# Blocks of the row maximum at moving slots, another set of units for GpSimd, and a held-back last tile

## The chip, the cores and the metric

The kernel runs on one core of a Trainium2 chip. Its metric is the device time of one execution in microseconds (us). The core has five engines, each with its own instruction queue: TensorE (PE in the rows; its weight loads are PEld) for matmuls, VectorE (DVE), ScalarE (ACT), GpSimd (POOL), and SyncE (SP), which here issues every DMA. The engines wait for each other only through semaphores. A matmul writes to PSUM, 8 banks of 2 KB for each of 128 partitions; the rest lies in SBUF.

## The reference

```
q: (4, 8, 1152, 64)   q_pool = mean of pairs of rows of q          -> (4, 8, 576, 64)
scores = q_pool @ k.T / 8;  attn = softmax(scores);  x = attn @ v   -> 2304 tokens x 512
h = x @ w_in (512 x 2048);  g = h * sigmoid(h);  y = g @ w_out
a = y @ w1;  b = y @ w2 (512 x 1024);  out = ((a * b) @ w3) @ w_out2
```

All in float32. The kernel makes each product from two parts of each operand, a high half rounded to the matmul's format and a low half (the value minus its high half): hi x hi + hi x lo + lo x hi, three matmuls for one.

## The kernel before

**Attention.** 32 heads are worked on as 16 pairs (index p in the code). The two heads of a pair lie on partitions 0 to 63 and 64 to 127, and TensorE issues their 64-row matmuls by twos, which run side by side. The text calls two such matmuls a slot. The keys of a pair are 9 chunks of 128, the queries two halves of 288, so a pair has 18 units u: 0 to 8 (half A) and 9 to 17 (half B). n = 18 p + u counts units through. For each unit TensorE computes the transposed scores (score_t, four slots, the last of which subtracts the row maximum), ScalarE takes the exponential twice (line 526 gives the high half pH, line 531 or 533 the full value), and VectorE (line 735) or GpSimd (line 442) subtracts the one from the other: this is the low half of the unit, pL. For a unit in POOL_UNITS it is made by GpSimd, from a copy in SBUF; else by VectorE, straight from PSUM. Then TensorE multiplies with v, two units later: values(n, 0) and values(n, 1), three slots each. So a unit has ten slots.

score_t(n) overwrites the PSUM banks of unit n - 2: it waits for the low half of unit n - 2, if VectorE makes it, and otherwise only for ScalarE's second exponential. values(n, 0) always waits for the low half of unit n.

**The maximum.** The row maximum of the next pair is found under the units of this one. The scores in their other layout are made in 15 blocks (score_max, line 925: three slots, 384 columns wide), VectorE reduces each (take_max, line 701). From pair 1 on, all blocks use one double bank, so a block waits for take_max of the block before. Blocks stand in units 17 and 0, 2 to 9 and 11 to 15; units 1, 10 and 16 have none. At the end reduce_max, negate and nine small matmuls (turn_max, line 936, in unit 17) turn the maximum.

**The order in a unit of TensorE**, written out by hand: scores; values(n - 3, 1); the block; values(n - 2, 0). In units 2 and 11 the block comes ahead of the scores, and there is no values(n - 3, 1), since units 1 and 10 do values(n - 3, 1), values(n - 2, 0), scores, values(n - 2, 1). In units 0, 9 and 17 the block stands at the end.

**The order in a unit of VectorE**: take_max of the block of unit u - 1; in units 2 and 11 take_o (lines 745, 746), which copies the finished sums of the half before out of PSUM and which values(.., 0) of the new half waits for; the low half of unit n - 1, if it is VectorE's; then what is tied to a unit: the casts of v (v_hi, line 694), the cast of a slice of w_in (w_hi, line 739), guard_sums and recip on the packed sums of the softmax. SP stores these sums to packed (pack_sums) and spreads their reciprocals (spread_rsums), GpSimd multiplies with them (normalize). GpSimd also makes the low halves of k, v, q and w_in (k_lo, v_lo, q_lo, w_lo). Each queue is in order.

**The two feed-forward parts** run in five tiles of 512 tokens, the last one of 256. In the second part a tile has eight chunks c: first2(t, c), 24 matmuls into two banks; then ScalarE copies one (aS), VectorE multiplies (pr, line 889), ScalarE takes the high half (prH), VectorE the low half (prL, line 892); second2(t, c), 12 matmuls, adds the chunk into four banks. TensorE's order is first2(c), second2(c - 1). At the end take_out copies the four banks to oS (lines 667, 880) and SP stores them.

Of the kernel before, what the change touches and what calls it, by code (L numbers as in the profile page):

```python
# [19 lines left out]
ALU = mybir.AluOpType  # L20
# [14 lines left out]
def block_kernel(nc, kT, qT, v, w_in, w_out, w1, w2, w3T, w_out2, consts_in, outT, recips):  # L35
# [26 lines left out]
    POOL_UNITS = (0, 3, 6, 9, 12, 15, 16)  # L62
# [14 lines left out]
    with ctx:  # L77
# [161 lines left out]
        out_taken = sem("out_taken")  # L239
        out_stored = [sem(f"out_stored{r}") for r in range(2)]  # L240
# [11 lines left out]

        def width(t):

            return slice(0, min(TILE, TOK - t * TILE))

        LO_POOL = len(POOL_UNITS) * PAIRS
        LO_DVE = ALL - LO_POOL

        def by_pool(n):  # L260

            return n % UNITS in POOL_UNITS

        def pool_order(n):

            return n // UNITS * len(POOL_UNITS) + sum(1 for u in POOL_UNITS if u < n % UNITS)
# [39 lines left out]
        def _(sp):  # L306
# [68 lines left out]
            for c in range(C1):  # L375
                if c == 1:
                    sp.wait_ge(pv_done, 2 * ALL)
                if c == 2:
                    pack_sums(PAIRS - 1)
                    spread_rsums(PAIRS - 1)  # L380
# [21 lines left out]
            for t in range(TILES):  # L402
                sp.wait_ge(out_taken, (t + 1) * MC)
                sp.dma_start(out_v[:, :, span(t)], oS[t % 2][:, :, width(t)]).then_inc(out_stored[t % 2], 16)
            for e in range(2):
                sp.wait_ge(out_stored[e], 16 * len(range(e, TILES, 2)))
# [3 lines left out]
        def _(pool):  # L410
# [71 lines left out]
            for p in range(PAIRS):  # L482
                first, more, more2 = p == 0, p + 1 < PAIRS, p + 2 < PAIRS
                n = UNITS * p
                p_lo(n)
                if more:
                    k_lo(p + 1, 2)
                if not first:
# [3 lines left out]
                p_lo(n + 3)  # L492
# [15 lines left out]
                if more2:  # L508
                    k_lo(p + 2, 1)
                p_lo(n + 15)  # L510
                p_lo(n + 16)
                if more:
                    v_lo(p + 1, 0)
            normalize(PAIRS - 1, 1, lo_done(ALL - 2))
# [5 lines left out]
        def _(act):  # L520
# [148 lines left out]
            def tile2(t, e, last):  # L669
                for c in range(C2):  # L670
# [3 lines left out]
                    w = width(t)  # L674
                    act.copy(aS[r][:, w], abbank[r][0][:, w]).then_inc(a_copied, 1)  # L675
                    act.wait_ge(pr_done, n + 1)
                    need(act, pr_used, n - 1)
                    act.copy(prH[r][:, w], pr[r][:, w]).then_inc(prH_ready, 1)
# [7 lines left out]
            take_out(TILES - 1, (TILES - 1) % 2)  # L686
# [3 lines left out]
        def _(dve):  # L690
# [126 lines left out]

# [342 lines left out]
```

## Time and profile before

| | us |
|---|---|
| median of 3 runs | 1308.18 (1308.13 to 1309.52) |
| the profiled execution | 1308.44 |
| its span on the core | 1306.6 |
| TensorE busy | 1294.4 (99%) |
| TensorE's weight loads busy | 1157.4 (89%) |
| VectorE busy | 606.8 (46%) |
| ScalarE busy | 581.1 (44%) |
| GpSimd busy | 366.7 (28%) |

The span is what lies between the first and the last instruction; 1.8 us lie around it. The granted clock of TensorE is full in all slices of the page. Attention takes the first 567 us. Matmul records overlap: a record begins when the matmul is taken up and not when its data streams, so the distance between the starts of two records tells more than their length.

### The profile page before, as it was taken

What the parts mean: (1) busy time and instruction counts of PE and PEld (TensorE: products, weight loads), DVE (VectorE), ACT (ScalarE), POOL (GpSimd) and SP (SyncE); (2) the same over time, 40 slices, a digit from 0 to 9 for tenths busy, and PEclk for the clock granted to TensorE, in tenths of its full rate; (3) what the DMA queues carried; (4) which work ended last, traced back from release to release, by engine and by line L of the source; (5) the groups of instructions that cost most, each with busy time, mean ns of one, the idle gap of its engine ahead of it and who ended that gap; (6) DMA issues with size and microseconds to landing.
All of it is one profiled execution on the core that took longest, in us unless ns stands there. A gap on an engine that the chain in (4) does not pass through costs nothing.

```text
span 1306.6 us, 26221 instructions
## 1 busy us (share of the span) xinstructions
PE 1294.4 (99%) x10980; PEld 1157.4 (89%) x10980; DVE 606.8 (46%) x934; ACT 581.1 (44%) x1050; POOL 366.7 (28%) x313
## 2 busy tenths in 40 slices
PE   8999999999999999999999999999999999999998
PEld 7999999999999999988888888888998888888888
DVE  6777777877777777533212112111146222222221
ACT  3666667666666666753322222222245212121111
POOL 4566666666666766520000000000000000000000
PEclk9999999999999999999999999999999999999999
DMA  4212222222222211011100000000043000000000
GB/s 139 65 59 69 74 74 73 74 74 74 74 73 74 73 55 38 19 51 49 32 1 1 1 1 1 1 1 32 18 158 117 1 1 33 1 33 1 33 18 31
DMA packets 25990, 58.59 MB, mean 45 GB/s; under 512 B 7184, under 2 KB 8720, under 8 KB 25872
## 3 DMA queue, kind: packets, MB, share of 16 engines
q1 hardware_dynamic: 25872, 56.91, 13.6%
q8 instruction: 87, 1.43, 0.4%
q14 instruction: 31, 0.25, 0.1%
HBM read 52.04 MB, written 4.79 MB: 43 GB/s over the span
## 4 chain that ended last, share of the span: by engine, by line
PE 98%; DVE 1%; DMA 0%; issue 0%; POOL 0%; ACT 0%; SPq 0%; DVEq 0%; POOLq 0%
PE psum L908 19%; PE psum L909 19%; PE psum L910 19%; PE psum L975 18%; PE psum L925 10%; PE psum L954 9%; PE psum L956 3%; DVE mx L701 1%; PE psum L936 1%; DMA kraw<-in_kT 0%; POOL kL L428 0%; PE psum L985 0%; DVE tmpB L746 0%; POOL qsum L470 0%; SPq L346 0%
## 5 line engine op out<-in xcount | busy, mean ns | idle before, releaser
L701 DVE TENSOR_REDUCE mx<-psum 128x2 f32<-128x768 f32 x240 | 228.6, 957 | 88.2 <-PE psum L925 88.2
L526 ACT ACTIVATE pH<-psum 128x576 fp32r<-128x576 f32 x288 | 188.1, 653 | 167.2 <-PE psum L956 164.1
L442 POOL TENSOR_TENSOR pL<-pF,pH 128x576 fp32r<-128x576 f32 x112 | 159.9, 1428 | 161.3 <-ACT pF L531 161.3
L845 DVE TENSOR_TENSOR gL<-gF,gH 128x512 fp32r<-128x512 f32 (+1 forms) x80 | 51.3, 641 | 306.1 <-ACT gH L606 306.0
L975 PE MATMUL psum<-pH,vH 64*128 64x288 f32 x1152 | 188.5, 300 | 1.5 <-DVE tmpB L746 1.0
L975 PE MATMUL psum<-pH,vL 64*128 64x288 f32 x1152 | 184.1, 292 | 0.0
L975 PE MATMUL psum<-pL,vH 64*128 64x288 f32 x1152 | 183.4, 291 | 0.0
L603 ACT ACTIVATE gF<-psum 128x512 f32<-128x512 f32 (+1 forms) x80 | 44.4, 555 | 267.1 <-PE psum L910 267.1
L735 DVE TENSOR_TENSOR pL<-psum,pH 128x576 fp32r<-128x576 f32 x176 | 132.1, 751 | 13.4 <-ACT psum L533 13.2
L975 PEld LDWEIGHTS psum<-pH,vH 64*128 64x128 f32 x1152 | 122.7, 185 | 8.0 <-issue 6.0
L975 PEld LDWEIGHTS psum<-pH,vL 64*128 64x128 f32 x1152 | 122.4, 184 | 0.0
L975 PEld LDWEIGHTS psum<-pL,vH 64*128 64x128 f32 x1152 | 122.3, 184 | 0.0
L889 DVE TENSOR_TENSOR pr<-aS,psum 128x512 f32<-128x512 f32 (+1 forms) x40 | 25.4, 634 | 201.6 <-ACT aS L675 201.6
L908 PE MATMUL psum<-xH,winH 128*128 128x512 f32 (+1 forms) x320 | 117.8, 368 | 0.3 <-PE psum L975 0.3
L908 PE MATMUL psum<-gH,woH 128*128 128x512 f32 (+1 forms) x320 | 117.9, 368 | 0.0
L910 PE MATMUL psum<-xH,winL 128*128 128x512 f32 (+1 forms) x320 | 117.7, 368 | 0.0
L909 PE MATMUL psum<-gL,woH 128*128 128x512 f32 (+1 forms) x320 | 117.7, 368 | 0.0
L910 PE MATMUL psum<-xH,w12L 128*128 128x512 f32 (+1 forms) x320 | 117.7, 368 | 0.0
L909 PE MATMUL psum<-xL,winH 128*128 128x512 f32 (+1 forms) x320 | 117.7, 368 | 0.0
L909 PE MATMUL psum<-xL,w12H 128*128 128x512 f32 (+1 forms) x320 | 117.7, 368 | 0.0
L910 PE MATMUL psum<-gH,woL 128*128 128x512 f32 (+1 forms) x320 | 117.7, 368 | 0.0
L908 PE MATMUL psum<-xH,w12H 128*128 128x512 f32 (+1 forms) x320 | 117.7, 368 | 0.0
(101 smaller groups left out, 2801.1 us busy)
## 6 DMA issues: line engine op xcount, KB each, us to landing
vraw<-in_v SPq DMA_DIRECT2D x16, 576.0 KB, 3.7
qraw<-in_qT SPq DMA_DIRECT2D x15, 576.0 KB, 4.7
kraw<-in_kT SPq DMA_DIRECT2D x15, 576.0 KB, 3.8
rsums<-recips SPq DMA_DIRECT2D x32, 144.0 KB, 3.0
wstage<-in_w_in SPq DMA_DIRECT2D x16, 256.0 KB, 4.6
fstage<-in_w3T SPq DMA_DIRECT2D x8, 512.0 KB, 4.6
w12stage<-in_w SPq DMA_DIRECT2D x8, 512.0 KB, 4.8
outT<-oS SPq DMA_DIRECT2D x4, 1024.0 KB, 4.1
```

Of the source, the lines that this page charges most:

```text
L442: pool.tensor_tensor(pL[r][:], pF[pool_order(n) % 2][:], pH[r][:].bitcast(F32), ALU.subtract).then_inc(pL_pool, 1)
L526: act.activation(pH[r][:], scores, ACT.Exp, scale=SCALE).then_inc(pH_ready, 1)
L603: act.activation(gF[:, w], hbank[r][:, w], ACT.Silu).then_inc(silu_done, 1)
L701: dve.tensor_reduce(mx[:, qt, :, kb], bank[:, :, 0:KW], AX.X, ALU.max).then_inc(max_taken, 1)
L735: dve.tensor_tensor(pL[r][:], stbank[n % 2], pH[r][:].bitcast(F32), ALU.subtract).then_inc(pL_dve, 1)
L845: dve.tensor_tensor(gL[r][:, w], gF[:, w], gH[r][:, w].bitcast(F32), ALU.subtract).then_inc(gL_ready, 1)
L908: pe.matmul(out, lhs_hi, rhs_hi, start=start, stop=False)
L909: pe.matmul(out, lhs_hi, rhs_lo, start=False, stop=False)
L910: return pe.matmul(out, lhs_lo, rhs_hi, start=False, stop=stop)
L925: last = pe.matmul(bank[:, hd, 0:KW], q[j][own(hd), cols], k[j][own(hd), keys], start=(s == 0), stop=(s == 2))
L954: pe.matmul(out[:, hd, :], k[j][own(hd), keys], r[j][own(hd), q], start=(s == 0), stop=False)
L975: last = pe.matmul(obank[hd], vals[own(rows_of), c, hd:hd + 2, :].rearrange("p e d -> p (e d)"), probs[own(rows_of), hd, :], start=(c == 0 ...
```

## The change

- **Blocks.** A table BLOCK_AT gives each block a slot: 0 is ahead of the scores, 4 behind them, 5 and 6 inside values(n - 3, 1), 7 behind it, 8 and 9 inside values(n - 2, 0), 10 the end of the unit. Units 3 to 9 have 4 to 10, units 12 to 15 have 4 to 7, units 2 and 11 have 0, units 17 and 0 have 10. Before, units 3 to 8 and 12 to 15 all had 7.
- **GpSimd's units** are 1, 4, 7, 10, 13, 15 and 16 of each pair, for 0, 3, 6, 9, 12, 15 and 16. The low half of the last pair's unit 16 goes to VectorE. GpSimd's order is written anew: the third k_lo goes ahead of the first low half, the second normalize ahead of the low half of unit 13, one k_lo to the end.
- **VectorE's casts.** v_hi(p, 1) moves from unit 1 to 2, v_hi(p, 2) from 4 to 5, w_hi from 7 to 8, guard_sums from 6 to 5, recip from 7 to 6.
- **Last sums later.** guard_sums and recip of the last pair move behind the first low half of g; SP spreads the reciprocals one chunk later. TensorE no longer waits for all of pv_done ahead of the first feed-forward product.
- **Last tile.** second2(6th chunk, c = 5) is held back behind first2 of the last chunk. Since the last tile is half as wide, prH and prL give four lanes there (lane, lane_free). The four sums are copied and stored by twos, each as soon as it is complete.

```diff
-    POOL_UNITS = (0, 3, 6, 9, 12, 15, 16)
+    BLOCK_AT = {17: 10, 0: 10, 2: 0, **{s: s + 1 for s in range(3, 10)}, 11: 0, **{s: s - 8 for s in range(12, 16)}}
+    POOL_UNITS = (1, 4, 7, 10, 13, 15, 16)
...
-            return n % UNITS in POOL_UNITS
+            return n % UNITS in POOL_UNITS and n != ALL - 2
...
-                    if u == 1 and not first:
+                    if u == 2 and not first:
                         v_hi(p, 1)
-                    if u == 4:
+                    if u == 5:
                         v_hi(p, 2)
+                    if u == 5 and not first:
+                        guard_sums(p - 1)
                     if u == 6 and not first:
-                        guard_sums(p - 1)
-                    if u == 7 and not first:
                         recip(p - 1)
-                    if u == 7:
+                    if u == 8:
                         w_hi(p)
...
+            def block_here(item, at, slot):
+
+                if item is not None and at == slot:
+                    score_max(*item)
+
...
-                    if u % NC == LAG and item is not None:
-                        score_max(*item)
-                    score_t(p, u)
+                    at = BLOCK_AT.get(u, 10)
+                    block_here(item, at, 0)
+                    score_t(p, u, item, at)
+                    slot = 4
                     if u == UNITS - 1 and p + 1 < PAIRS:
                         turn_max(p + 1)
+                    block_here(item, at, slot)
                     if u % NC != LAG and n > LAG:
-                        values(n - LAG - 1, 1)
-                    if u % NC not in (0, LAG) and u != UNITS - 1 and item is not None:
-                        score_max(*item)
+                        values(n - LAG - 1, 1, item, at, slot)
+                        slot += 3
+                        block_here(item, at, slot)
                     if n >= LAG:
-                        values(n - LAG, 0)
+                        values(n - LAG, 0, item, at, slot)
+                        slot += 3
...
             pe.wait_ge(winH_ready, PAIRS)
             pe.wait_ge(winL_ready, PAIRS)
-            pe.wait_ge(pv_done, 2 * ALL)
...
             def tile2(t, e):
                 for c in range(C2):
                     first2(t, e, c)
+                    if t == TILES - 1 and c == C2 - 2:
+                        continue
+                    if t == TILES - 1 and c == C2 - 1:
+                        second2(t, c - 2)
                     if c > 0:
                         second2(t, c - 1)
```

GpSimd's order in a pair, before and after:

```diff
-                p_lo(n)
                 if more:
                     k_lo(p + 1, 2)
+                p_lo(n + 1)
...
-                p_lo(n + 3)
+                p_lo(n + 4)
...
-                p_lo(n + 6)
+                p_lo(n + 7)
                 w_lo(p)
-                p_lo(n + 9)
+                p_lo(n + 10)
...
-                    normalize(p - 1, 1, (qL_ready, 2 * (p + 2) + 1) if more2 else lo_done(n + 9))
-                p_lo(n + 12)
+                    normalize(p - 1, 1, (qL_ready, 2 * (p + 2) + 1) if more2 else lo_done(n + 10))
+                    normalize(p - 1, 0, (normalized, 2 * p - 1))
+                p_lo(n + 13)
                 if more2:
                     k_lo(p + 2, 0)
-                if not first:
-                    normalize(p - 1, 0, (normalized, 2 * p - 1))
+                p_lo(n + 15)
+                if by_pool(n + 16):
+                    p_lo(n + 16)
+                if more:
+                    v_lo(p + 1, 0)
                 if more2:
                     k_lo(p + 2, 1)
```

## Rows read from the trace of the kernel before

**Rows 1.** Chain's shares by engine; one pair's length, busy PE, PEld, DVE, ACT, POOL
```profile
PE 98%; DVE 1%; DMA 0%; issue 0%; POOL 0%; ACT 0%; SPq 0%; DVEq 0%; POOLq 0%
...
300.00:334.23 34.23, 34.21 (x464) 33.06 (x462) 26.92 (x42) 23.63 (x43) 22.91 (x20) 1.00 0.21 70
```

**Rows 2.** Timeline of TensorE (start, length, engine, line): first and last in-pair turn
```profile
55.77 0.64 PE L936 MATMUL psum<-identR,mneg 64*128 64x64 f32 x9
...
535.01 0.64 PE L936 MATMUL psum<-identR,mneg 64*128 64x64 f32 x9
```

**Rows 3.** Timelines of TensorE and VectorE, half B, units 13, 14: blocks, take_max
```profile
254.45 0.44 PE L925 MATMUL psum<-kH,qH 64*128 64x384 f32 x2
...
255.05 0.32 PE L975 MATMUL psum<-pH,vH 64*128 64x288 f32 x2
...
256.38 0.44 PE L925 MATMUL psum<-kH,qH 64*128 64x384 f32 x2
...
255.28 0.96 DVE L701 TENSOR_REDUCE mx<-psum 128x2 f32<-128x768 f32 x1 [0.98 <-PE psum L925]
```

**Rows 4.** Timeline of TensorE, next pair's half A: units 2 and 3
```profile
266.80 0.35 PE L925 MATMUL psum<-kH,qH 64*128 64x384 f32 x2
...
268.20 0.32 PE L975 MATMUL psum<-pH,vL 64*128 64x288 f32 x2
...
268.91 0.29 PE L954 MATMUL psum<-qH,kL 64*128 64x288 f32 x2
```

**Rows 5.** Timeline of VectorE in the same units: take_o, low half, take_max, low half
```profile
267.03 0.46 DVE L745 COPY tmpA<-psum 128x288 f32<-128x288 f32 x1 [0.31 <-PE psum L975]
267.40 0.45 DVE L746 COPY tmpB<-psum 128x288 f32<-128x288 f32 x1
267.86 0.76 DVE L735 TENSOR_TENSOR pL<-psum,pH 128x576 fp32r<-128x576 f32 x1
268.53 0.95 DVE L701 TENSOR_REDUCE mx<-psum 128x2 f32<-128x768 f32 x1
```

**Rows 6.** Casts (ns min/median/max), one beside GpSimd, stores to packed (us to landing)
```profile
L694 DVE CAST vH<-vraw x46: 537/541/547, 31.7 to 542.7; 128x384 fp32r<-128x384 f32 x46
...
L739 DVE CAST winH<-wstage x16: 366/980/1110, 37.5 to 547.5; 128x512 fp32r<-128x512 f32 x16
...
277.28 0.99 DVE L739 CAST winH<-wstage 128x512 fp32r<-128x512 f32 x1
...
276.55 1.43 POOL L442 TENSOR_TENSOR pL<-pF,pH 128x576 fp32r<-128x576 f32 x1 [1.96 <-ACT pF L531]
...
packed<-tmpB SPq DMA_DIRECT2D x16, 2.2 KB, 3.3
```

**Rows 7.** Timelines, half B: unit 11's block on TensorE, second exp on ScalarE
```profile
249.68 0.36 PE L925 MATMUL psum<-kH,qH 64*128 64x384 f32 x2
...
251.51 0.65 ACT L533 ACTIVATE psum<-psum 128x576 f32<-128x576 f32 x1
```

**Rows 8.** Timelines at attention's end: TensorE, and GpSimd's last two low halves
```profile
564.77 0.40 PE L975 MATMUL psum<-pH,vH 64*128 64x288 f32 x2
...
567.05 0.29 PE L975 MATMUL psum<-pL,vH 64*128 64x288 f32 x2
...
567.94 0.39 PE L909 MATMUL psum<-xL,winH 128*128 128x512 f32 x1
...
561.90 2.82 POOL L442 TENSOR_TENSOR pL<-pF,pH 128x576 fp32r<-128x576 f32 x2 [1.33 <-ACT pF L531]
```

**Rows 9.** Timelines and DMA list at the end: TensorE, VectorE's last copies, last store
```profile
1300.14 0.28 PE L910 MATMUL psum<-prH,foldL 128*128 128x256 f32 x1
1300.80 0.39 PE L908 MATMUL psum<-prH,foldH 128*128 128x256 f32 x1 [0.38 <-DVE prL L892]
...
1302.54 0.76 DVE L880 COPY oS<-psum 128x256 f32<-128x256 f32 x2 [1.79 <-PE psum L910]
...
outT<-oS SPq DMA_DIRECT2D x1, 512.0 KB, 2.9
```

More of the change, by code:

```diff
@@ L673, in tile2 @@
                     need(act, pr_done, n - 1)
[L674 removed]
+                    w, into = width(t), lane(t, c)
                     act.copy(aS[r][:, w], abbank[r][0][:, w]).then_inc(a_copied, 1)
                     act.wait_ge(pr_done, n + 1)
[L677 to L678 removed]
+                    need(act, pr_used, lane_free(t, c))
+                    act.copy(prH[r][:, into], pr[r][:, w]).then_inc(prH_ready, 1)
                     if c == C2 // 2 and not last:
@@ L685, in _ @@
                 tile2(t, t % 2, t == TILES - 1)
-            take_out(TILES - 1, (TILES - 1) % 2)
+            need(act, out_stored[(TILES - 1) % 2], 8 * (TILES - 1 - (TILES - 1) % 2))
+            for m in range(0, MC, 2):
+                act.wait_ge(last_summed, m + 1)
+                act.copy(oS[(TILES - 1) % 2][:, m, width(TILES - 1)], accbank[m][:, width(TILES - 1)]).then_inc(last_act, 1)
         @block.vector
@@ L815, in _ @@
             take_o(PAIRS - 1, 1)
-            guard_sums(PAIRS - 1)
-            recip(PAIRS - 1)
             def take_y(t):
@@ L848, in tile1 @@
                         take_y(t - 1)
+                    if c == 0 and first:
+                        guard_sums(PAIRS - 1)
+                        recip(PAIRS - 1)
                     if last and c == C1 - 3:
@@ L900, in _ @@
                 tile2(t, t % 2, t == TILES - 1)
-            take_out(TILES - 1, (TILES - 1) % 2)
+            need(dve, out_stored[(TILES - 1) % 2], 8 * (TILES - 1 - (TILES - 1) % 2))
+            for m in range(1, MC, 2):
+                dve.wait_ge(last_summed, m + 1)
+                dve.tensor_copy(oS[(TILES - 1) % 2][:, m, width(TILES - 1)], accbank[m][:, width(TILES - 1)]).then_inc(last_dve, 1)
         @block.tensor
@@ L957, in score_t, with values @@
                               ).then_inc(st_scored, 1)
-            def values(n, part):
+            def values(n, part, item=None, at=None, first_slot=0):
                 p, u = n // UNITS, n % UNITS
@@ L1020, in _ @@
                         pe.wait_ge(m_placed_odd, p + 2)
-                    if (u % NC == 0 or u == UNITS - 1) and item is not None:
+                    if item is not None and at >= slot:
                         score_max(*item)
@@ L1043, in first1, with second @@
                 last.then_inc(h_ready, 1)
-            def second(hi, lo, w, wH, wL, c, chunks):
+            def second(hi, lo, w, into, wH, wL, c, chunks, each=None):
                 for m in range(MC):
                     cols = slice(m * P, (m + 1) * P)
-                    last = three(accbank[m][:, w], wH[:, c, cols], wL[:, c, cols], hi[:, w], lo[:, w],
+                    last = three(accbank[m][:, into], wH[:, c, cols], wL[:, c, cols], hi[:, w], lo[:, w],
                                  start=(c == 0), stop=(c == chunks - 1))
+                    if each is not None:
+                        last.then_inc(each, 1)
                 return last
@@ L1112, in second2 @@
                         pe.wait_ge(foldL_ready, C2)
-                second(prH[c % 2], prL[c % 2], width(t), foldH, foldL, c, C2).then_inc(pr_used, 1)
+                if (t, c) == (TILES - 1, C2 - 1):
+                    second(prH[c % 2], prL[c % 2], lane(t, c), width(t), foldH, foldL, c, C2, last_summed)
+                else:
+                    second(prH[c % 2], prL[c % 2], lane(t, c), width(t), foldH, foldL, c, C2).then_inc(pr_used, 1)
             def tile2(t, e):
```

47 lines of the change are left out of this document (32 added, 15 removed).

## The prediction

> **What bounds the kernel now.** I read the chain of work that ended last first: its shares by engine put 98% on TensorE [rows 1]. So every other engine counts only where TensorE waits for it. The table of one pair's stretch says how much that can be: in 34.23 us TensorE is recorded busy for 34.21, but its weight loads for 33.06, VectorE for 26.92, ScalarE for 23.63, GpSimd for 22.91 [rows 1]. The matmul column hides short waits, since a matmul's record begins before it streams. The wait shows as a longer distance between starts. So I read TensorE's timeline by start-to-start distance. Two turns of the maximum, 14 pairs apart, are (535.01 - 55.77) / 14 = 34.23 us per pair [rows 2]. Undisturbed, ten slots take 1.33 us, as from 255.05 to 256.38 [rows 3], 0.132 or 0.133 each; a block is three slots of 384 columns instead of 288, 3 x 0.132 x 384 / 288 = 0.53. A full unit is 1.85 us.
>
> The waits of a pair, from those rows:
>
> - Units four to eight and 13 to 15 each begin their block with a first pair recorded 0.44 instead of 0.35 us (that of 266.80 did not wait), and the next block starts 1.93 us on, not 1.85 [rows 3, 4]. It is a loop: the block must wait for take_max of the block before (one bank). A take_max that starts at 255.28 ends at 256.24, and the block's true start is 0.22 after that, 256.46 [rows 3]. From one true start to the next: block 0.53, 0.23 to take_max, 0.96, 0.22, together **1.94 us**. Ten slots and a block give 1.85. Price 0.08, eight times a pair: 0.64.
> - Unit 2 and unit 11. Block at 266.80 (0.53), scores (0.53), then the unit's values could stream at 267.86. They wait for take_o: VectorE copies at 267.03 and 267.40, to 267.85 [rows 5]; the second pair at 268.20 says that streaming began at 268.07 [rows 4]. Price 0.21 to 0.23, twice.
> - Unit 3 and unit 12. Its scores could stream at 268.07 + 0.395 = 268.46, but wait for the low half of unit 1 (VectorE 267.86, ends 268.62 [rows 5]); the second pair at 268.91 puts the true start at 268.78 [rows 4]. Price 0.31, twice: 0.62.
>
> **The change, part by part.**
>
> *Blocks at slots of their own.* Units 3 to 9 and 12 to 15 have 11 slots between blocks: 0.53 + 11 x 0.132 = 1.98 us against the loop's 1.94. The eight waits of 0.08 go, with only 0.04 us to spare: gain 0.64. The block of unit 0 still follows that of unit 17 by ten slots and keeps its wait.
>
> *GpSimd's units rotate.* Units 1 and 10 go to GpSimd. TensorE's scores two units later then need only ScalarE's second exp, which had ended by 267.86, when VectorE's low half of unit 1 began [rows 5]: both 0.31 go, gain 0.62. Units 0, 3, 6, 9, 12 come to VectorE, 2, 5, 8, 11, 14 stay. Unit 0's low half fits between take_max of block 0 and take_o at 267.03, where the cast of v stood. GpSimd keeps seven low halves a pair and is 33% idle.
>
> *The price in half A.* The cast of v now stands behind take_o in unit 2. Where row 267.86 has the low half, VectorE runs the cast: 0.54 us [rows 6], 0.46 start to start (the low half of 0.76 us is 0.67 start to start, 267.86 to 268.53 [rows 5]). take_max of unit 2's block starts 268.32, ends 269.28, so unit 3's block streams from 269.50. In the new order that block stands behind the scores alone, at 268.46 + 0.53 = 268.99. **Wait of 0.51 us**, in pairs 1 to 14. Before, it was due at 268.78 + 0.53 + 0.40 = 269.71, and take_max of 268.53 let it at 268.53 + 0.95 + 0.22 = 269.70: no wait [rows 5]. take_max follows at 270.26, the loop of the later blocks has its 1.98 again.
>
> *The price in half B.* No cast there. Counted from the block of unit 11 at 249.68 [rows 7]: take_o ends 1.05 later, take_max runs 250.74 to 251.69, unit 12's block could stream at 251.88 and may at 251.91: 0.03. But the low half of unit 11 needs the second exp, 251.51 to 252.16 [rows 7]; it runs 252.25 to 253.00 and holds take_max of unit 12 from 252.67 to 252.92, end 253.88. Unit 13's block, due at 252.44 + 0.79 + 0.53 + 0.13 = 253.89, streams at 254.10: 0.21. Together 0.24.
>
> Per pair: 0.64 + 0.62 - 0.51 - 0.24 = **0.51 us**; pairs 1 to 14 give 7.1. Pair 0 has neither the cast nor take_o of an earlier pair, and its unit 4 block waits some 0.3 more: gain 0.3. Pair 15 has no blocks; there the 0.31 of units 3 and 12 go and the other waits for low halves move: gain 0.6, bounds 0 and 1.
>
> *What is moved and costs nothing.* guard_sums a unit earlier: the two stores to packed follow take_o (267.85), about 0.5 us of issue each, and the later lands 3.3 us after its issue [rows 6], near 272.2; guard_sums comes up near 273.6 (take_max of unit 4's block and the cast before it). If that cover were gone, VectorE, and behind it take_max, would stand for the rest. GpSimd's queue: both normalize now stand before the low half of unit 13; at about 1.43 us each [rows 6] I count that low half 1.4 us later than its exp allows, and its values are due 1.2 us after it. SP's queue: load_k waits for k_lo(p+1, 2), which now goes before a low half instead of behind one, so it is earlier; load_v waits for v_lo(p, 2), one unit later, with ten units left.
>
> *The cast of w_in, and a rule.* It took 366 ns once and 980 in the middle [rows 6]: started at 277.28 it ended 0.3 us after GpSimd's low half (276.55 + 1.43) [rows 6]. In unit 8 it meets the low half of unit 7, ends near 280.13, and take_max of that unit's block is due at 280.18: nothing, with 0.05 to spare. The Trainium skill ("SBUF — State Buffer", Who interferes with whom) says that a VectorE cast in a two-port mode and a GpSimd instruction exclude each other for a whole instruction, and that the later one blocks; by that rule, the trace agrees for this cast. It speaks against the change at the other cast, that of v, which would now start beside GpSimd's low half of unit 1; what that would do is the third rival.
>
> *Attention's end.* The low half of unit 16 leaves GpSimd, whose two run to 564.72, for VectorE; begun when GpSimd began, at 561.90 + 1.41 = 563.31, it ends by 564.1 with 0.76 us; its values began at 564.77, right behind GpSimd's end, with a first record of 0.40 [rows 8]. GpSimd's end without waits of its own was 0.6 us later than VectorE's would be; TensorE's earlier work caps what is won. Bounds 0 and 0.6, taken 0.2. TensorE then no longer waits for pv_done: last values at 567.05, next could stream at 567.18, streamed at 567.94 - 0.23 = 567.71 [rows 8]. Gain 0.5; late next could be xL, which VectorE writes one chunk after the other behind unit 17's low half, so the bounds are 0 and 0.5. The last sums are packed and read later under matmuls; their first use is eight chunks on: nothing.
>
> *The last tile.* The order first2(7), second2(6), second2(7) leaves the chain through aS, pr, prH, prL open: 1300.14 + 0.12 to 1300.91 = 0.65 [rows 9]. With second2(5) and second2(6) both behind first2(7), 2.9 us cover it. The copies go out by bank: VectorE's two took 0.76 and one is 0.42, so the last ends 0.34 sooner [rows 9]. The last store carries 256 KB for 512, whose landing took 2.9 [rows 9]; no row has 256 KB here; bounds 0 and 1.45 (half of the 2.9, if it all scaled), taken 0.3, nearer to none, since its twin is in flight until shortly before. Gain 1.3.
>
> Sum: 7.1 + 0.3 + 0.6 + 0.2 + 0.5 + 1.3 = **10.0 us**. The profiled execution took 1308.44, 0.26 above the median of 1308.18. 1308.18 - 10.0 = **1298.2 us**.
>
> **The rivals.**
>
> 1. *Unit 3 does not wait for the cast.* If VectorE gets to take_max in time, 14 x 0.51 = 7.1 come on top: 1291. For it: nothing but my ordering; against it: VectorE works in order in every row, and the code has the cast first.
> 2. *The loop keeps its waits.* The spare 0.04 us is less than a twentieth of one take_max. If an operation between (the low half held by its exp, guard_sums, recip) pushes each take_max by 0.1, the 0.08 stays at all eight blocks: 15 x 0.64 = 9.6 back: 1307.8, no change. For it: unit 13 already shows such a push. Against: elsewhere the low half ends 0.4 us before the next take_max.
> 3. *The cast of v blocks behind GpSimd: slower.* In unit 2 it starts at 267.86, GpSimd's low half of unit 1 at about 267.9. Were it held as the cast of w_in is, it would end at 267.93 + 1.43 + 0.28 = 269.64 and unit 3's block stream at 270.72, 1.22 later than forecast: 14 x 1.22 = 17.1, time 1315.3. It decides from 0.71 us a pair on. Against: 46 casts of v took 537 to 547 ns [rows 6], under whatever GpSimd did; the one beside the low half of unit 0 too.
> 4. *Only the ends do anything*, the pairs giving zero: 1308.2 - 2.6 = 1305.6, at the edge of what counts as no change. It is between 2 and the forecast.
>
> **How the numbers follow.** Forecast within 3 us: 0.60. Rival 1: 0.14. Rivals 2 and 4: 0.14, half of it wholly, half in a milder form. Rival 3: 0.05. Anything else: 0.07, spread over the signs. The likeliest is the forecast, 1298.2. The range reaches down to rival 1 (1291) and up to where half of the eight waits stay (1298.2 + 4.8 = 1303): 1290.5 to 1303.5. This kernel's measurement tells 0.2%, 2.6 us, from no change. Faster 0.85 (0.60 + 0.14, the mild half of rivals 2 and 4, and 0.04 of the rest), same 0.08, slower 0.07.
>
> **What would show it.** Right: turns 33.7 us apart; first pairs of blocks in units 4 to 8 at 0.35 to 0.37; no wait of unit 3's scores; in half A the block of unit 3 half a microsecond late behind take_max, with a 0.54 us cast before it; unit 13's block 0.2 late; last store issued about 1 us nearer to the last product. Wrong: blocks still at 0.44 (rival 2), the cast of v above 1 us (rival 3), GpSimd's low halves late for values, or a new wait at unit 10 or 11 for VectorE, which now has unit 9 before take_o with 0.1 us to spare.

## The result and the profile after

| | before | after |
|---|---|---|
| median, us | 1308.22 (6 runs, 1308.12 to 1309.73) | 1296.41 (6 runs, 1295.50 to 1296.55) |
| the profiled execution, us | 1308.44 | 1295.50 |
| its span, us | 1306.6 | 1293.7 |
| turn of the maximum to turn, us per pair | 34.23 | 33.50 |

The ratio is 0.9904, 95% interval [0.9892, 0.9917]; 1298.2 was predicted. The two profiled executions differ by 12.94 us, and it is these that are accounted for below; the medians differ by 11.81, as four of the six executions of after are 0.9 us above its profiled one (the experiments with idle matmuls are about that) and before's median is 0.22 under its own.

The page of the changed kernel, with VectorE's largest group, take_max (busy and mean ns, then idle time before it and its releaser):

```profile
PE 1281.0 (99%) x10980; PEld 1150.8 (89%) x10980; DVE 616.6 (48%) x935; ACT 581.1 (45%) x1050; POOL 365.2 (28%) x312
...
L726 DVE TENSOR_REDUCE mx<-psum 128x2 f32<-128x768 f32 x240 | 228.4, 956 | 72.0 <-PE psum L953 70.2
```

TensorE's busy time fell by 13.4 us although it computes the same: a matmul's record begins before its data streams and so holds part of its wait, and the fall is waiting. VectorE's busy time rose by 9.8 us; nearly all of that is no extra work either: 8.1 us are in guard_sums (14 of its 16 records are 0.58 longer) and 1.1 in the casts of w_in (16.4 for 15.3), both below.

The same table of one pair as in [rows 1], and the first and last turn as in [rows 2]:

```profile
300.00:333.50 33.50, 33.37 (x463) 32.64 (x461) 27.53 (x42) 23.62 (x43) 22.92 (x19) 1.00 0.24 72
```

```profile
55.44 0.65 PE L964 MATMUL psum<-identR,mneg 64*128 64x64 f32 x9
...
524.43 0.68 PE L964 MATMUL psum<-identR,mneg 64*128 64x64 f32 x9
```

(524.43 - 55.44) / 14 = 33.50 us per pair: 0.73 less than before, times 14 is 10.25 of the 12.94 us. The first turn comes 0.33 earlier (55.77 before); last turn to first streaming feed-forward product takes 556.40 - 524.43 = 31.97 for 32.70: 0.73 (the stream's start is the second product's record, 556.63, less one product of 0.23). The rest, 1.63, lies in the feed-forward part.

TensorE in units 2 and 3 of half A, which answers to [rows 4]; L1012 is values, L989 and L991 the scores, L953 the block:

```profile
262.98 0.34 PE L991 MATMUL psum<-mrow,selR 64*128 64x288 f32 x2
263.27 0.40 PE L1012 MATMUL psum<-pH,vH 64*128 64x288 f32 x2
...
263.60 0.33 PE L1012 MATMUL psum<-pL,vH 64*128 64x288 f32 x2
263.73 0.34 PE L989 MATMUL psum<-qH,kH 64*128 64x288 f32 x2
...
264.13 0.33 PE L991 MATMUL psum<-mrow,selR 64*128 64x288 f32 x2
...
264.84 0.37 PE L953 MATMUL psum<-kL,qH 64*128 64x384 f32 x2
```

Two things are to be seen. The scores of unit 3 follow the values in step (263.60, 263.73): the 0.31 us wait for a low half is gone. And unit 3's block, due at 264.13 + 0.13 = 264.26, has its second pair at 264.84, so it streamed from 264.66: a new wait of 0.40 us. The wait for take_o is still there (values due at 263.11, streaming from 263.60 - 0.26 = 263.34: 0.23).

VectorE (take_o L770, L771; v_hi L719; take_max L726; low half L760; guard_sums L775) in the same pair, as [rows 5]:

```profile
262.67 0.45 DVE L771 COPY tmpB<-psum 128x288 f32<-128x288 f32 x1
263.04 0.54 DVE L719 CAST vH<-vraw 128x384 fp32r<-128x384 f32 x1
263.50 0.95 DVE L726 TENSOR_REDUCE mx<-psum 128x2 f32<-128x768 f32 x1
...
268.74 0.75 DVE L775 TENSOR_SCALAR packed<-packed 128x9 f32<-128x9 f32 x1
269.40 0.95 DVE L726 TENSOR_REDUCE mx<-psum 128x2 f32<-128x768 f32 x1
```

take_max ends at 264.45 and the block streams 0.21 later. GpSimd beside it (low halves at 263.18 and 268.02), and the groups of v_hi, w_hi and guard_sums (ns min/median/max), as [rows 6]:

```profile
263.18 1.42 POOL L464 TENSOR_TENSOR pL<-pF,pH 128x576 fp32r<-128x576 f32 x1 [1.30 <-ACT pF L553]
...
268.02 1.43 POOL L464 TENSOR_TENSOR pL<-pF,pH 128x576 fp32r<-128x576 f32 x1 [1.69 <-ACT pF L553]
```

```profile
L719 DVE CAST vH<-vraw x46: 538/542/546, 33.8 to 533.6; 128x384 fp32r<-128x384 f32 x46
L764 DVE CAST winH<-wstage x16: 417/1064/1066, 39.7 to 537.8; 128x512 fp32r<-128x512 f32 x16
L775 DVE TENSOR_SCALAR packed<-packed x16: 163/744/747, 67.7 to 561.2; 128x9 f32<-128x9 f32 x16
```

The row of guard_sums in the kernel before:

```profile
L750 DVE TENSOR_SCALAR packed<-packed x16: 162/164/174, 70.5 to 570.9; 128x9 f32<-128x9 f32 x16
```

All 46 casts of v take what they took before, the one inside GpSimd's low half too. But guard_sums, nine elements, took 164 ns at the median before and takes 744 now. In the 14 pairs in which it begins inside a low half of GpSimd it takes 733 to 747 ns; the two times when no GpSimd instruction runs beside it, it takes 163 and 168. Two experiments below are about that.

Unit 13's block in half B (VectorE's low half of unit 11, which waits for ScalarE and holds up take_max; then TensorE), which answers to [rows 7]:

```profile
281.35 0.76 DVE L760 TENSOR_TENSOR pL<-psum,pH 128x576 fp32r<-128x576 f32 x1 [0.59 <-ACT psum L555]
```

```profile
282.88 0.33 PE L1012 MATMUL psum<-pH,vH 64*128 64x288 f32 x2
...
283.37 0.36 PE L953 MATMUL psum<-kL,qH 64*128 64x384 f32 x2
```

Due at 283.01, streaming from 283.37 - 0.18 = 283.19: 0.18 late. Unit 12's block does not wait. In units 2 to 15 of this pair, only this block and unit 3's have a first record above 0.40.

The ends, as [rows 8] and [rows 9]: TensorE in the last pair and at the handover, TensorE's last product, and the last two stores:

```profile
549.99 0.40 PE L1012 MATMUL psum<-pH,vH 64*128 64x288 f32 x2 [0.15 <-POOL pL L464]
...
556.07 0.29 PE L1012 MATMUL psum<-pL,vH 64*128 64x288 f32 x2
...
556.63 0.40 PE L937 MATMUL psum<-xL,winH 128*128 128x512 f32 x1
```

```profile
1290.23 0.28 PE L938 MATMUL psum<-prH,foldL 128*128 128x256 f32 x1
```

```profile
outT<-oS SPq DMA_DIRECT2D x2, 256.0 KB, 2.2
```

The last pair has a wait that was not there before: the values of 549.99, due at 549.66, stream from 550.09 (their second pair is recorded at 550.22), 0.43 late, for a low half of GpSimd. The first feed-forward product streams at 556.40, possible were 556.20. The last product to the span's end is 1293.7 - 1290.23 = 3.47 us; before it was 4.38.

### The profile page after: what moved, and what is told of

The parts are those of the page before. It is cut to its first block, busy times and chain, and to the rows that moved or that the text cites. A ratio compares the mean times of both kernels' runs of the same rounds, so it can differ in the third digit from the quotient of the medians.

```text
span 1293.7 us, 26208 instructions
## 1 busy us (share of the span) xinstructions
PE 1281.0 (99%) x10980; PEld 1150.8 (89%) x10980; DVE 616.6 (48%) x935; ACT 581.1 (45%) x1050; POOL 365.2 (28%) x312
## 4 chain that ended last, share of the span: by engine, by line
PE 97%; DVE 1%; issue 0%; POOL 0%; DMA 0%; ACT 0%; SPq 0%; POOLq 0%; DVEq 0%
PE psum L936 19%; PE psum L937 19%; PE psum L938 19%; PE psum L1012 18%; PE psum L953 10%; PE psum L989 9%; PE psum L991 3%; DVE mx L726 1%; PE psum L964 1%; DMA kraw<-in_kT 0%; POOL kL L450 0%; ACT pH L548 0%; POOL pL L464 0%; POOL xT L478 0%; PE psum L1022 0%
## 5 line engine op out<-in xcount | busy, mean ns | idle before, releaser
L726 DVE TENSOR_REDUCE mx<-psum 128x2 f32<-128x768 f32 x240 | 228.4, 956 | 72.0 <-PE psum L953 70.2
L1012 PE MATMUL psum<-pH,vH 64*128 64x288 f32 x1152 | 186.8, 300 | 1.6 <-DVE tmpB L771 1.0
L1012 PE MATMUL psum<-pH,vL 64*128 64x288 f32 x1152 | 182.8, 292 | 0.0
L1012 PE MATMUL psum<-pL,vH 64*128 64x288 f32 x1152 | 182.6, 292 | 0.0
L760 DVE TENSOR_TENSOR pL<-psum,pH 128x576 fp32r<-128x576 f32 x177 | 132.8, 750 | 25.9 <-ACT psum L555 24.0
L1012 PEld LDWEIGHTS psum<-pH,vH 64*128 64x128 f32 x1152 | 121.0, 185 | 8.3 <-issue 5.1
L1012 PEld LDWEIGHTS psum<-pH,vL 64*128 64x128 f32 x1152 | 120.7, 185 | 0.0
L1012 PEld LDWEIGHTS psum<-pL,vH 64*128 64x128 f32 x1152 | 120.6, 185 | 0.0
```

The costliest lines, as they stand in the source:

```text
L726: dve.tensor_reduce(mx[:, qt, :, kb], bank[:, :, 0:KW], AX.X, ALU.max).then_inc(max_taken, 1)
L760: dve.tensor_tensor(pL[r][:], stbank[n % 2], pH[r][:].bitcast(F32), ALU.subtract).then_inc(pL_dve, 1)
L1012: last = pe.matmul(obank[hd], vals[own(rows_of), c, hd:hd + 2, :].rearrange("p e d -> p (e d)"), probs[own(rows_of), hd, :], start=(c == 0 ...
```

## The experiments

Every kernel is the changed one with the edit shown. The ratio is that to the kernel before, run on the same chip.

| | median, us | ratio, 95% interval | turns, us |
|---|---|---|---|
| the changed kernel | 1296.41 | 0.9904 [0.9892, 0.9917] | 33.50 |
| old_slots | 1297.14 | 0.9914 [0.9901, 0.9928] | 33.62 |
| old_units | 1308.18 | 0.9998 [0.9989, 1.0007] | 34.33 |
| cast_unit1 | 1294.52 | 0.9892 [0.9878, 0.9905] | 33.37 |
| cast_unit17 | 1292.67 | 0.9880 [0.9866, 0.9893] | 33.27 |
| cast17_slots | 1289.35 | 0.9851 [0.9838, 0.9865] | 33.06 |
| ends_undone | 1296.99 | 0.9908 [0.9894, 0.9921] | 33.50 |
| guard_unit6 | 1303.29 | 0.9958 [0.9943, 0.9973] | 34.00 |
| cast_even | 1295.82 | 0.9902 [0.9886, 0.9919] | 33.53 |
| cast17_busy | 1292.22 | 0.9872 [0.9859, 0.9886] | 33.27 |
| after_busy | 1295.78 | 0.9897 [0.9883, 0.9910] | 33.50 |
| best | 1289.06 | 0.9847 [0.9834, 0.9860] | 33.07 |

### old_slots: the blocks back at slot 7

```diff
-    BLOCK_AT = {17: 10, 0: 10, 2: 0, **{s: s + 1 for s in range(3, 10)}, 11: 0, **{s: s - 8 for s in range(12, 16)}}
+    BLOCK_AT = {17: 10, 0: 10, 2: 0, **{s: 7 for s in range(3, 9)}, 9: 10, 11: 0, **{s: 7 for s in range(12, 16)}}
```

> The changed kernel with the blocks back at their old slots (7 in units 3 to 8 and 12 to 15); GpSimd's new units, the casts and the ends stay. By the loop of 1.94 us (block, take_max, block) against ten slots and a block of 1.85: first pairs of the blocks in units 4 to 8 and 13 to 15 are recorded 0.44 us again, eight waits of 0.08 come back (0.64 a pair), while the waits of units 3 (0.40) and 13 (0.18) of the changed kernel go: 0.06 a pair more, turns 33.56 apart, about 1 us over the changed kernel, 1297.5. Rival, that the slots make the gain and the units are only their companions: turns near 34.2, about 1307.

Measured 33.62 a pair. TensorE's blocks of units 5 and 6 in this kernel:

```profile
267.42 0.44 PE L953 MATMUL psum<-kH,qH 64*128 64x384 f32 x2
...
269.36 0.44 PE L953 MATMUL psum<-kH,qH 64*128 64x384 f32 x2
```

The 0.44 records and the 1.94 us loop are back in eight blocks, and the waits of units 3 and 13 are gone: behind three and two more slots their take_max had ended. Eight waits of 0.08 are 0.64, the two that they replace 0.40 + 0.18 = 0.58; that net of 0.06 is half of the 0.12 measured. The averages over pairs 1 to 14 say where the rest is: from its last score slot to the next unit's, a unit of these eight takes 1.942 us here, and 1.852 in the changed kernel where its block does not wait. That is 0.09 each, 0.72 for eight, and 0.72 - 0.58 = 0.14. So the moving slots, beside the new units, are worth 0.12 us a pair, not 0.64: most of what they win they pay at once, as two of the blocks that now come early wait.

### old_units: GpSimd's units and the casts as before, new slots kept

```diff
-    POOL_UNITS = (1, 4, 7, 10, 13, 15, 16)
+    POOL_UNITS = (0, 3, 6, 9, 12, 15, 16)
...
-                    if u == 2 and not first:
+                    if u == 1 and not first:
                         v_hi(p, 1)
...
```

(GpSimd's order and the units of the other casts, of guard_sums and of recip go back likewise, so what follows holds for all of these together.)

> The changed kernel with GpSimd's units 0, 3, 6, 9, 12, 15, 16, its old order and VectorE's casts and guard_sums at their old units; the new slots and the ends stay. By my sum: the eight waits of 0.08 stay away, the waits of units 3 and 12 for VectorE's low half of units 1 and 10 are back (0.31 each), and the block of units 3 and 12, now right behind the scores, is due at 2.51 us after unit 2's block and may start at 2.90: 0.39 each. Turns 34.23 - 0.64 + 0.78 = 34.37 apart, that is slower than before in the pairs; with 2 to 3 us from the ends about 1307.5. Rival, that slots and units each give their share: turns 34.23 - 0.64 = 33.6, about 1297.

Measured 34.33. TensorE's scores and block of unit 3:

```profile
268.79 0.32 PE L1013 MATMUL psum<-pL,vH 64*128 64x288 f32 x2
269.13 0.40 PE L990 MATMUL psum<-qH,kH 64*128 64x288 f32 x2
...
270.08 0.44 PE L954 MATMUL psum<-kH,qH 64*128 64x384 f32 x2 [0.17 <-DVE mx L727]
```

The scores wait 0.31 us for the low half, and then the block, three slots earlier than it was, another 0.40 for take_max behind that same low half; unit 12 is alike. The new slots by themselves cost 0.10 a pair against the kernel before; the new units by themselves gain 34.23 - 33.62 = 0.61; together they gain 0.73. The two parts are not a sum: the slots pay only where the low halves have left units 3 and 12.

### cast_unit1 and cast_unit17: the cast of v out of unit 2

The first has `if u == 1` for `if u == 2` ahead of v_hi(p, 1). The second takes the cast into the pair before:

```diff
                         v_hi(p + 1, 0)
                         place_odd(p + 1)
+                        v_hi(p + 1, 1)
...
-                    if u == 2 and not first:
-                        v_hi(p, 1)
```

> The changed kernel with the cast of v (second third) back in unit 1, in front of take_o instead of behind it. By queue order: the cast starts where VectorE's low half of unit 0 leaves off, 0.05 us after unit 2's block, and take_o starts 0.28 later; unit 2's values wait 0.28 longer, unit 3's block does not wait any more (was 0.40): 0.12 a pair less, turns 33.38 apart, 1294.7. If the wait of unit 3's block has nothing to do with the cast, it stays at 0.40 and the time grows by 14 x 0.28 = 3.9 us to 1300.

> The changed kernel with the same cast moved into unit 17 of the pair before, behind place_odd, where VectorE stands idle for 1.08 us. By queue order: unit 3's block no longer waits (0.40), but take_max of unit 3's block is then held by the low half of unit 2, which waits for ScalarE, as in half B, so unit 4's block waits 0.18: net 0.22 a pair, turns 33.28 apart, 14 x 0.22 = 3.1 us less, 1293.3. Rival: the cast delays take_max of unit 17's block or waits for pv_done there; then unit 0's block starts later and the gain is lost, 1296.4 or more.

Measured 33.37 and 33.27. TensorE in cast_unit1, then in cast_unit17, same pair:

```profile
263.54 0.40 PE L1012 MATMUL psum<-pH,vH 64*128 64x288 f32 x2 [0.22 <-DVE tmpB L771]
...
264.40 0.33 PE L991 MATMUL psum<-mrow,selR 64*128 64x288 f32 x2
264.54 0.37 PE L953 MATMUL psum<-kH,qH 64*128 64x384 f32 x2
```

```profile
263.91 0.33 PE L990 MATMUL psum<-mrow,selR 64*128 64x288 f32 x2
264.04 0.37 PE L952 MATMUL psum<-kH,qH 64*128 64x384 f32 x2
...
266.12 0.46 PE L952 MATMUL psum<-kH,qH 64*128 64x384 f32 x2
```

In both, unit 3's block follows its scores in one slot. That shows that the 0.40 us wait was the cast's. In unit 1 the cast pushes take_o instead (values of unit 2 wait 0.49 for 0.23), in unit 17 it pushes nothing, and what comes next late is unit 4's block, 0.18 us, behind a low half that waits for ScalarE. 0.40 removed, 0.23 gained a pair.

### cast17_slots: that wait given room

cast_unit17, with each block one more slot later where it can be:

```diff
-**{s: s + 1 for s in range(3, 10)}, 11: 0, **{s: s - 8 for s in range(12, 16)}}
+**{s: min(s + 2, 10) for s in range(3, 10)}, 11: 0, **{s: s - 7 for s in range(12, 16)}}
```

> cast_unit17 with the blocks one slot later: 5 to 10 in units 3 to 8, 10 in unit 9, 5 to 8 in units 12 to 15. There the low half of unit 2 (and 11) holds take_max of the next block by 0.18 to 0.2 us behind its due time; a block one slot (0.13) later loses only 0.04. Units 8 and 9 then both have slot 10 and stand ten slots apart: one wait of 0.08 is back; and the turn of the maximum waits 0.07 for a later last block. Per pair 0.12 instead of 0.18 in half A, 0.11 instead of 0.18 in half B: turns 33.27 - 0.13 = 33.14, 15 x 0.13 = 2 us less, 1290.7. Rival: the later last block delays reduce_max, negate and the turn by its whole 0.13 and more; then nothing is left of it.

Measured 33.06 for 33.14 expected. Three waits of 0.03 to 0.07 remained in the pair that was read. It says that the waits of units 4 and 13 were a matter of one slot of 0.13 us.

### ends_undone: the last tile's order and the wait for pv_done put back

```diff
+            pe.wait_ge(pv_done, 2 * ALL)
...
-                    if t == TILES - 1 and c == C2 - 2:
-                        continue
-                    if t == TILES - 1 and c == C2 - 1:
-                        second2(t, c - 2)
```

> The changed kernel with both ends undone: TensorE waits for pv_done again ahead of the first feed-forward product, and second2 of chunk 5 of the last tile is no longer held back (the stores by halves stay). My sum has 0.5 for the first; by the changed kernel's own trace (last values at 556.07, first product streaming at 556.40 where 556.20 was possible) it is 0.33. The second: 0.65, the open chain through aS, pr, prH, prL. Together 1.0: 1297.4. Turns stay 33.50 apart. Rival: the chain was hidden anyway or the first product waits for xL; then one of the two shows no difference in the trace.

Span 1294.7 for 1293.7. TensorE at the handover and in the last tile:

```profile
556.96 0.40 PE L937 MATMUL psum<-xL,winH 128*128 128x512 f32 x1
```

```profile
1289.16 0.28 PE L938 MATMUL psum<-prH,foldL 128*128 128x256 f32 x1
1289.82 0.39 PE L936 MATMUL psum<-prH,foldH 128*128 128x256 f32 x1 [0.38 <-DVE prL L917]
```

The product streams at 556.73 for 556.40, 0.33 us later, and the stall of 0.65 (1289.82 + 0.11 for 1289.16 + 0.12) is back: together the 1.0 us of the spans.

### guard_unit6: guard_sums one unit later

```diff
-                    if u == 5 and not first:
+                    if u == 6 and not first:
                         guard_sums(p - 1)
```

> guard_sums one unit later, in unit 6, the rest as in the changed kernel. In the changed kernel it starts at 268.74 beside GpSimd's low half (268.02 + 1.43 = 269.45) and is recorded 0.744 us for 9 elements; in the kernel before it took 0.164. Theory H (it is held until the GpSimd instruction beside it has ended): in unit 6 it starts behind the low half of 270.27, near 270.93, beside GpSimd's normalize (270.38 + 1.44 = 271.82), is recorded 0.9 us, and take_max of 271.38 starts near 271.78, so unit 7's block comes 0.4 less the spare 0.04 later: 0.36 a pair, turns 33.86 us apart, median near 1301.4. Rival N (0.744 belongs to unit 5, to its data or to the cast ahead of it): 0.16 us, turns 33.50, 1296.4.

Measured 34.00 a pair, 1303.29. VectorE, GpSimd, and TensorE's block of unit 7 (L779 is recip). The GpSimd instruction that the expectation calls normalize is sum_q, which adds the pairs of rows of q:

```profile
274.91 0.93 DVE L775 TENSOR_SCALAR packed<-packed 128x9 f32<-128x9 f32 x1
275.88 0.21 DVE L779 RECIPROCAL packed<-packed 128x9 f32<-128x9 f32 x1
```

```profile
274.38 1.44 POOL L436 TENSOR_TENSOR qsum<-qraw 128x576 f32<-128x576 f32 x1
```

```profile
276.45 0.30 PE L1012 MATMUL psum<-pH,vH 64*128 64x288 f32 x2
...
277.30 0.37 PE L953 MATMUL psum<-kL,qH 64*128 64x384 f32 x2
```

guard_sums ends at 275.84, 0.02 after GpSimd's 275.82, as theory H has it. recip must wait for guard_sums and stands ahead of take_max; that 0.13 was not in the expected 0.36, and the wait is 0.54 (due 276.58, streaming from 277.12), which leaves 0.05 open. So it goes in 13 of the pairs 1 to 14 (13 x 0.54 / 14 = 0.50, the turns). In pair 14 GpSimd has no sum_q left to do, nothing runs beside guard_sums, and it takes 165 ns; this is the same instruction in the same unit. An instruction of 9 elements costs this kernel 0.5 us in each pair, 6.9 us in all, by standing one unit later.

### cast_even: the cast of v in another walk

```diff
-                dve.tensor_copy(vH[:, vpiece(j), 0:3:2, :],
-                                vraw[:, vpiece(j), :].rearrange("p c (e d) -> p c e d", e=2)).then_inc(vH_ready, 1)
+                dve.tensor_copy(vH[:, vpiece(j), 0:3:2, :].rearrange("p c e d -> p e c d"),
+                                vraw[:, vpiece(j), :].rearrange("p c (e d) -> p e c d", e=2)).then_inc(vH_ready, 1)
```

> VectorE's casts of v walk their 3 x 2 x 64 elements as 2 x 3 x 64 (the two heads outermost), the rest as in the changed kernel; same elements, same units. Theory P (a VectorE copy from SBUF to SBUF is held by GpSimd only where it runs in its faster mode, and the casts of v, 542 ns for 384 elements, do not, while those of w_in, 417 ns for 512, and guard_sums do; the odd 3 in front is what keeps them out of it): from 163 ns for 9 and 417 for 512 elements the cast takes near 0.35 us alone. In unit 2 it starts 0.14 us ahead of GpSimd's low half (263.04 against 263.18), so it goes first and wins 0.2 of the 0.40 wait; in unit 5 it starts at 268.28 inside GpSimd's low half (268.02 to 269.45) and is held to about 269.7, guard_sums behind it, take_max of 269.40 starts 0.3 to 1.3 late. Together turns between 33.6 and 34.6, median 1298 to 1312, records of the cast from 350 to above 1400 ns. Rival C (faster and never held): turns 33.3, median 1293.6. Rival S (the walk does not matter): 542 ns, 1296.4.

The two groups of cast_even, v_hi and guard_sums, then VectorE in units 2 and 5 and GpSimd beside them:

```profile
L719 DVE CAST vH<-vraw x46: 347/351/1384, 33.8 to 534.0; 128x384 fp32r<-128x384 f32 x46
...
L775 DVE TENSOR_SCALAR packed<-packed x16: 162/163/168, 68.3 to 561.7; 128x9 f32<-128x9 f32 x16
```

```profile
263.17 0.35 DVE L719 CAST vH<-vraw 128x384 fp32r<-128x384 f32 x1
...
268.23 1.38 DVE L719 CAST vH<-vraw 128x384 fp32r<-128x384 f32 x1
```

```profile
263.30 1.50 POOL L464 TENSOR_TENSOR pL<-pF,pH 128x576 fp32r<-128x576 f32 x1 [1.30 <-ACT pF L553]
...
267.97 1.42 POOL L464 TENSOR_TENSOR pL<-pF,pH 128x576 fp32r<-128x576 f32 x1 [1.42 <-ACT pF L553]
```

This is theory P. The same 384 elements take 0.35 us for 0.54 where nothing is in the way. In unit 2 the cast began ahead of GpSimd's low half, took its 0.35, and the low half was the one to lose, 1.50 for 1.42. In unit 5 it began inside a low half (to 269.39) and ended only at 269.61. So it goes in each of the 14 pairs that have both: 350 or 351 ns ahead of the low half, 1383 or 1384 inside it. Unit 3's block waits 0.2 less and unit 6's 0.2 more, so the turns are 33.53, just under the expected 33.6: guard_sums came clear of GpSimd this time, whose next piece waits for this cast.

### The idle matmuls: cast17_busy, after_busy, best

The executions of one kernel lie in two groups some 1 us apart: after had 1295.50 and 1295.55 at a mean granted clock of 1.000, the other four 1296.40 to 1296.55 at 0.998. The profiled execution of cast_unit17 was of the second group. Its table by stretches, then that of cast17_busy, which adds the edit below, idle matmuls about unit 1's block of the first pair (columns as [rows 1]; the granted clock stands behind POOL's, 0.52 in one row):

```diff
+                    if n == 1:
+                        keep_busy(6)
                     if item is not None and at >= slot:
                         score_max(*item)
+                    if n == 1:
+                        keep_busy(8)
```

```profile
20.00:27.90 7.90, 5.20 (x67) 4.47 (x66) 4.48 (x9) 3.20 (x7) 1.95 (x2) 1.00 0.03 4
27.90:31.30 3.40, 3.40 (x30) 3.40 (x31) 1.18 (x2) 1.45 (x3) 0.47 (x1) 0.52 0.48 169
```

```profile
27.90:31.30 3.40, 3.40 (x50) 3.32 (x48) 2.12 (x3) 2.39 (x5) 1.05 (x2) 1.00 0.40 156
```

> cast_unit17 with 14 slots of idle matmuls in pair 0 where TensorE stands still between units 0 and 2 (0.9 and 1.3 us, ahead of the blocks of units 1 and 2). In cast_unit17's profiled execution the granted clock is 0.52 in the 3.4 us behind these gaps, and that stretch takes 1.2 us longer than in the changed kernel's, where it is 1.00. If the gaps are what lets the clock fall, all executions keep 1.00 and the median falls by about 1 us, to 1291.7, without a second group of times 1 us up. If the clock falls for another reason, times and their two groups stay as they are.

> The changed kernel with the same 14 slots of idle matmuls in pair 0. Of its six timed executions four had a mean granted clock of 0.998 and took 1296.4 to 1296.6, two had 1.000 and took 1295.5. If TensorE's standing still in pair 0 lets the clock fall, all executions now have 1.000 and lie at 1295.5 to 1296. If not, about two thirds stay near 1296.5.

> cast17_slots with the idle matmuls of cast17_busy: the sum of the two, since one touches pairs 1 to 15 and the other only the start. Turns 33.05 apart, as in cast17_slots; all executions at clock 1.000, so 1289.0 to 1289.4 and no group at 1290.5. Rival: the idle matmuls cost time themselves, by holding back unit 1's or 2's block; then the fast group moves up by as much as they are late.

TensorE was recorded busy for 6.91 of the 7.90 us ahead in cast17_busy, for 5.20 in cast_unit17. The profiled executions of guard_unit6 and cast17_slots have the same dip in the same stretch (0.53 and 0.56, behind 5.20 and 5.18 us busy). Those of after and old_slots have none there, behind 5.19 and 5.20: what TensorE did ahead does not alone decide it. All four executions of cast17_busy and all five of best ran at 1.000 and within 0.55 us; after_busy lay at 1295.46 to 1296.00, one of four at 0.999 from another stretch (6 to 20 us, granted 0.88). The medians move by 0.3 to 0.6 us (cast17_busy by 0.45 where 1 was expected), which the intervals of the ratios don't part from nothing. So that the idle matmuls take the dip away rests on the clock of 13 executions, 12 of them at 1.000, against two of six for the changed kernel, and against 17 of 35 for the eight kernels of this document with the new units and without idle matmuls; among these old_slots had four of four, guard_unit6 none of four. It is likely and not shown.

best is cast17_slots with the idle matmuls: 1289.06 us, ratio 0.9847 [0.9834, 0.9860], 7.4 us under the changed kernel.

## Why the prediction was right, and where it was not

| step | predicted, us | measured, us |
|---|---|---|
| eight block waits of a pair | +0.64 | gone, +0.68 |
| scores of units 3 and 12 | +0.62 | gone, +0.60 |
| half A, unit 3's block behind the cast of v | -0.51 | -0.40 |
| half B, blocks of units 12 and 13 | -0.24 | -0.18 |
| one pair, turn to turn | +0.51 | +0.73 |
| pairs 1 to 14 | 7.1 | 10.25 |
| pair 0 | 0.3 | 0.33 |
| pair 15, attention's end, pv_done | 0.6 + 0.2 + 0.5 | 0.73 (0.33 of it pv_done) |
| last tile and store | 0.65 + 0.34 + 0.3 | 1.63 |
| sum | 10.0 | 12.94 |

- **The mechanism held.** The order of VectorE set unit 3's block, as the experiments that move the cast show; rival 1, in which that block would not wait, needed 33.2 a pair and is out.
- **Part of the closeness is luck.** The account is 2.9 us off and the median only 1.8 us off the forecast, since the lower clock in four of the six executions, which no term of the sum has, took some 0.9 us back. Within the account the last pair and the handover, over-estimated by 0.6, hide part of what the pairs were under-estimated by.
- **The terms mis-sized** are the two prices. In half A the cast starts 0.37 after the copy ahead of it begins, where 0.46 stood in my chain, and the block streamed 0.21 after take_max; 0.11 a pair, 1.5 us in all. In half B unit 12's 0.03 did not come and unit 13's 0.21 is 0.18: 0.8 us. With the measured prices the sum is 0.64 + 0.62 - 0.40 - 0.18 = 0.68. The remaining 0.05 a pair, 0.7 us, lies in the gains. Averaged over pairs 1 to 14, from its last score slot to the next unit's, each of the eight units took 1.937 us before and 1.852 after where its block does not wait: 0.085 each, 0.68 for 0.64. In the same way the two waits of the scores were 0.60, the prices are 0.39 and 0.18, and unit 12 is 0.02 shorter: together 0.73.
- **Rival 2** (the loop keeps its 0.08 with 0.04 us to spare) did not happen: seven of the eight blocks it named have no 0.44 record, and that of unit 13 is the wait of half B. But its reason was sound. In guard_unit6 one take_max starts at 276.01 and ends at 276.91; two before it lie 1.98 apart, which puts its end at 276.31. Of the push of 0.60 the block pays 0.54: the spare is 0.06.
- **Rival 3** (the cast of v held) is out, 46 of 46 casts took 538 to 546 ns. Its argument (46 casts that were never held) was right and did not say why: cast_even shows that the walk of the operands decides it. The rows held it already, since the cast of v takes 542 ns for 384 elements where that of w_in takes 366 for 512 [rows 6]: the one held was the one with the faster rate. The Trainium skill ("VectorE: DVE Perf Modes", What auto-detection actually checks) gives the condition of the two-port mode: a single source and destination in SBUF whose outermost dimensions are both even or equal. The source is walked as 3 x 128 that lie one behind the other. Taken as one run of 384 its outermost dimension is even and that of the destination, three pieces, is not; by that rule, the trace agrees, before and after the walk was changed. Taken as 3 x 128, both would be 3 and the first walk would be in the mode, against the trace; no run separates the merging of the source from the rest.
- **"guard_sums a unit earlier costs nothing"** was right with the wrong reason. I looked at when its input lands and not at what GpSimd does beside it. It is held to 269.49, and take_max of unit 5's block starts at 269.40, when it was due anyway. In the next unit it is not free: guard_unit6 costs 6.9 us. The rule on shared access that I applied to the cast ("SBUF — State Buffer", Who interferes with whom, in the Trainium skill) applies to it too; by that rule, the trace agrees (0.02 to 0.04 us from GpSimd's end to its own).
- **The cast of w_in**, forecast to cost nothing in unit 8, cost nothing: it is held as before (1.06 us, 0.29 past the end of GpSimd's low half), and no block of unit 8 or 9 waits.
- **Rival 4** is out: the ends gave 2.7 of the 12.94, the pairs 10.25.
- **The last pair and the handover** were over-estimated, 0.73 for 1.3. Of the pv_done wait 0.33 came and not 0.5: streaming still started 0.2 later than the values allow; what that waits for was not tested. I had put 0.6 on the last pair, in which GpSimd now has unit 13 behind a normalize; a wait of 0.43 for it appeared (the units of this pair have no blocks and are shorter; in the other pairs the same order makes no wait), and three waits of 0.36 near 553.40, 554.55 and 555.70 stayed. That is read from the trace, not tried.
- **The tail** was under-estimated. The stall of 0.65 came as sized. Copies and store together gave 4.38 - 3.47 = 0.91 for 0.64: the 256 KB store lands in 2.2 us where 512 KB took 2.9, so 0.7 where I had 0.3, and that leaves 0.2 for the copies, for which I had 0.34. The store alone was not tried.

## What to carry to other kernels

In a loop over one buffer, list for each step what stands between the reader and the next writer on the reader's engine; moving a step elsewhere helps only until the next such list is the longest, and here removing 0.7 us of waits gave back 0.58, removing 0.40 gave back 0.18. Two changes to the order can be worth 0.61 and -0.10 alone and 0.73 together, so try them apart and together. Before moving even a tiny VectorE instruction, look at which GpSimd instruction it will stand beside, and whether it is of the kind that is held: the sign is a fast rate per element and a maximum far above its minimum.

## What the runs showed of the hardware

- A VectorE copy, cast or tensor_scalar from SBUF to SBUF that lands inside a GpSimd instruction ends just after it, if it is of the kind that is held: 9 elements in 0.75 or 0.93 us for 0.163, 384 in 1.38 for 0.35. It ends 0.03 us after the GpSimd instruction with 9 elements, 0.22 with 384 and 0.29 with the 512 of w_in. Whether it is held depends on how the operands are walked: the same 384 elements as 3 x 2 x 64 take 0.54 us and are never held, as 2 x 3 x 64 take 0.35 and are. A reciprocal inside GpSimd's sum_q (270.93, in the changed kernel) took its 0.20.
- The one that starts first wins: with the cast 0.13 us ahead, GpSimd's low half took 1.50 us for 1.42, in 15 pairs of cast_even.
- The granted clock of TensorE was 0.52 for 3.4 us, near its lower level of 1.2 GHz, after it had been busy for 5.20 of 7.90 us (and stayed at 2.4 GHz after 5.19 of 7.90 in the profiled execution of the changed kernel); 30 records of matmuls lie in that stretch, 48 in the same stretch of the changed kernel. The whole cost is 1 us of 1296, and it came in some executions of a kernel and not in others.
- A block that waits for take_max streams 0.21 or 0.22 us after take_max's recorded end, at each place that was read.
